# An attention stage in front of two feed-forward networks: four steps a pair, reciprocals through DRAM, weight preparation spread

## The reference

```python
def _attn_ref(q, k, v, M_prev, z_prev, beta):
    scores = scale * np.matmul(q, k.transpose(0, 1, 3, 2))
    scores = np.where(causal, -1000000000.0, scores)
    a = np.exp(scores - scores.max(-1, keepdims=True))
    a /= a.sum(-1, keepdims=True) + 1e-09
    local = np.matmul(a, v)
    q_p = phi(q)                       # where(q > 0, q, exp(q) - 1) + 1
    mem_ret = np.einsum('bhsd,bhde->bhse', q_p, M_prev)
    mem_norm = np.einsum('bhsd,bhd->bhs', q_p, z_prev)[..., None] + 1e-06
    g = 1.0 / (1.0 + np.exp(-beta))[None, :, None, None]
    return g * (mem_ret / mem_norm) + (1 - g) * local

x = (silu(x @ w_gate) * (x @ w_val)) @ w_out
h = x @ w_in
x = np.where(h >= 1, h, np.where(h <= -1, 0.0, (h + 1) ** 2 / 4)) @ w_out2
```

## Time and profile before

| | us |
|---|---|
| median of three runs | 1084.59 (1083.61 to 1087.66) |
| the profiled execution | 1084.93 |
| its span | 1083.0 |
| TensorE busy, share of the span | 1011.7, 93% |
| DVE, ACT, POOL busy | 817.6, 572.6, 535.4 |

### The profile page before, as it was taken

One profiled execution on the slowest core, in us unless ns is written; L12 is line 12 of the kernel. 1 busy time (PEld: TensorE's weight loads), 2 busy tenths in 40 slices (PEclk: granted clock), 3 DMA queues, 4 the chain that ended last, 5 costly groups with the idle time before them and its releaser, 6 DMA issues.

```text
span 1083.0 us, 21225 instructions
## 1 busy us (share of the span) xinstructions
PE 1011.7 (93%) x6440; PEld 931.9 (86%) x6440; DVE 817.6 (75%) x1580; ACT 572.6 (53%) x1162; POOL 535.4 (49%) x455
## 2 busy tenths in 40 slices
PE   4698999899899989999899999999999999999998
PEld 2466666667899979999899999999999999999997
DVE  4567777787677867677766777888898879987876
ACT  3556666776644544454534445554464554654551
POOL 4645555565875843235622347655744325523321
PEclk9889999999999999999999999999999999999999
DMA  4212333312433322342223322232331432234211
GB/s 156 75 56 88 94 94 94 94 46 79 156 117 125 110 98 98 116 137 79 98 98 119 116 98 98 98 117 92 104 117 63 172 118 91 85 117 142 92 40 59
DMA packets 47662, 109.56 MB, mean 101 GB/s; under 512 B 11360, under 2 KB 21600, under 8 KB 47584
## 3 DMA queue, kind: packets, MB, share of 16 engines
q1 hardware_dynamic: 47584, 108.56, 29.9%
HBM read 93.86 MB, written 14.68 MB: 100 GB/s over the span
## 4 chain that ended last, share of the span: by engine, by line
PE 77%; DVE 7%; issue 6%; ACT 3%; POOL 3%; DMA 2%; SPq 1%; DVEq 1%; ACTq 0%; POOLq 0%
PE ps L1325 22%; PE ps L1327 21%; PE ps L1326 21%; PE ps L1301 4%; PE ps L1253 4%; PE ps L1272 4%; DVE xt_l L1049 1%; ACT rown L721 1%; DVE xy L1135 1%; DVE hid_r L1125 1%; DVE tmp L1119 1%; DMA zb<-z 1%; PE ps L1294 1%; ACT wu_h L771 1%; DMA wu_r<-w_up 1%
## 5 line engine op out<-in xcount | busy, mean ns | idle before, releaser
L634 POOL TENSOR_TENSOR wu_l<-wu_r,wu_h 128x768 fp32r<-128x768 f32 (+1 forms) x75 | 140.6, 1883 | 394.1 <-ACT wu_h L771 394.0
L1325 PE MATMUL ps<-xt_h,wu_h 128*128 128x384 f32 x840 | 282.7, 337 | 16.9 <-DVE xt_l L1049 10.2
L1327 PE MATMUL ps<-xt_h,wu_l 128*128 128x384 f32 x840 | 280.8, 334 | 0.0
L1326 PE MATMUL ps<-xt_l,wu_h 128*128 128x384 f32 x840 | 280.8, 334 | 0.0
L1325 PE MATMUL ps<-hid_h,wd_h 128*128 128x384 f32 x672 | 226.7, 337 | 7.5 <-DVE xy L1135 7.3
L1327 PE MATMUL ps<-hid_h,wd_l 128*128 128x384 f32 x672 | 225.3, 335 | 0.0
L1326 PE MATMUL ps<-hid_l,wd_h 128*128 128x384 f32 x672 | 225.2, 335 | 0.0
L1135 DVE TENSOR_TENSOR xy<-xy,ps 128x384 f32<-128x384 f32 x288 | 157.5, 548 | 57.0 <-PE ps L1327 56.0
L830 ACT ACTIVATE hid_h<-hid_r 128x768 fp32r<-128x768 f32 x84 | 70.9, 844 | 209.1 <-DVE hid_r L1109 153.8
L1325 PEld LDWEIGHTS ps<-xt_h,wu_h 128*128 128x128 f32 x840 | 157.6, 188 | 23.9 <-issue 23.3
L1326 PEld LDWEIGHTS ps<-xt_l,wu_h 128*128 128x128 f32 x840 | 157.7, 188 | 0.0
(11 more groups left out here) (75 smaller groups left out, 1401.3 us busy)
## 6 DMA issues: line engine op xcount, KB each, us to landing
wu_r<-w_up SPq DMA_DIRECT2D x60, 512.0 KB, 4.7
wd_r<-w_down SPq DMA_DIRECT2D x42, 512.0 KB, 3.5
wu_r<-kept SPq DMA_DIRECT2D x38, 512.0 KB, 5.5
kept<-wu_r SPq DMA_DIRECT2D x19, 512.0 KB, 4.5
qk<-qT SPq DMA_DIRECT2D x16, 288.0 KB, 2.8
qk<-kT SPq DMA_DIRECT2D x16, 288.0 KB, 3.1
qn<-q_rest SPq DMA_DIRECT2D x16, 256.0 KB, 2.9
vm<-v_rest SPq DMA_DIRECT2D x16, 256.0 KB, 3.2
```

The lines of the kernel that those rows point to most:

```text
L634: nc.gpsimd.tensor_tensor(wu_l[u % 3][:, a:b], wu_r[u % 3][:, a:b], wu_h[u % 2][:, a - 1:b - 1].bitcast(F32), ALU.subtract).then_inc(low_p ...
L1325: nc.tensor.matmul(dst, w_hi, v_hi, start=start, stop=False, skip_group_check=onto)
L1326: nc.tensor.matmul(dst, w_hi, v_lo, start=False, stop=False, skip_group_check=onto)
L1327: return nc.tensor.matmul(dst, w_lo, v_hi, start=False, stop=stop, skip_group_check=onto)
```

## The change

- Tiles 1 to 4 come in the order 4, 3, 2, 1, four steps a pair. The first 64 queries of both heads are one tile of 128 rows: a block diagonal matrix of the queries, prepared ahead, gives their scores in one matmul over 128 rows (scores_f), with its own mask, maximum and exp, in the step of tile 1. The distances are now MEMS 1, TURN 3, VALUES 5, EVAC 6; ROWN, NEGS and PTS fall from 5 to 4.
- The reciprocals of a whole pair are one operation of nine columns (sums_inverse). SP writes them to the DRAM tensor rsums, turned (write_r), waits until they are there, and issues four reads that broadcast them over 64 partitions each (read_r). DVE multiplies from there in two pieces a pair. POOL's copies, TensorE's transposes and ACT's copies of reciprocals are gone.
- Three loads a pair in place of eight: qk_in (Q, K and the block diagonal), nat_in (q by rows, z beside it), vm_in (M_prev and V). qk_in of pair 0 is the first of all.
- No loop: all steps are written out, and no register is counted.
- wu_r2, wu_l2 and wu_h1 have a place of their own. The loads of weight steps 0 to 2 are issued at the start; their sums, high and low parts and the X parts stand at single steps of the attention (SUMS_AT and the tables beside it).
- The copies of groups to pt: one of nine is on DVE, before three of nine.

```diff
-    ROWN, NEGS, PTS = 5, 5, 5
+    EXP, MEMS, TURN, VALUES, EVAC = 1, 1, 3, 5, 6
+    ROWN, NEGS, PTS = 4, 4, 4
+    SUMS_AT, LOW_AT, HIGH_AT = (34, 38, 45), (42, 47), (38, 43)
+    KEEP = 11
+    X_SUMS_AT = (46, 48, 50, 52)
+    X_HIGH_AT = (48, 50, 52, 54, 56, 58, 60)
...
+            def write_r(p):
+                sp.wait_ge(rdend, p + 1)
+                sp.dma_start(rsums[p].rearrange("b p -> p b"), rden[:, p % 2], allow_slow_non_contiguous=True).then_inc(r_out, 16)
+
+            def read_r(p):
+                sp.wait_ge(r_out, 16 * (p + 1))
+                at_least(sp, x_done, 2 * (p - 1))
+                for h in range(2):
+                    half = slice(D * h, D * h + D)
+                    first = rsums[p, 0:1, half].broadcast_to([D, D])
+                    sp.dma_start(rbc[half, p % 2, 0:D], first).then_inc(r_in[p % 2], 16)
+                    rest = rsums[p, 1:].rearrange("(o i h) n -> o i h n", o=1, h=2)[:, :, h]
+                    sp.dma_start(rbc[half, p % 2, D:].rearrange("p (i n) -> p i n", n=P),
+                                 rest.broadcast_to([D, SLOTS, P])).then_inc(r_in[p % 2], 16)
...
+            for p in range(1, NPAIR):
+                if p + 1 < NPAIR:
+                    load_qk(p + 1)
+                    load_nat(p + 1)
+                write_r(p - 1)
+                if p > 1:
+                    load_v(p)
+                read_r(p - 1)
+                if p == KEEP:
+                    keep_sums(1)
...
+            def sums_inverse(p):
+                at_least(dve, expd, 2 * SLOTS * (p + 1))
+                at_least(dve, expdf, p + 1)
+                nc.vector.tensor_scalar(den[:, p % 2], rsum[:, p % 2], 1e-9, None, ALU.add).then_inc(dend, 1)
+                at_least(dve, dend, p + 1)
+                at_least(dve, r_out, 16 * (p - 1))
+                nc.vector.reciprocal(rden[:, p % 2], den[:, p % 2]).then_inc(rdend, 1)
...
             def out_x(j):
+                p, i = tile_of(j)
+                if i not in (3, 1):
+                    return
+                at_least(dve, pv_done, j + 1)
+                at_least(dve, r_in[p % 2], 64 * (p // 2 + 1))
+                dst, o, r = x_part(p, 0 if i == 3 else 1)
                 nc.vector.tensor_tensor(dst, o, r, ALU.mult).then_inc(x_done, 1)
...
+            def scores_f(j):
+                p, i = tile_of(j)
+                if i > 1:
+                    return
+                s = p % 2
+                at_least(pe, maxed, 2 * j - 1)
+                nc.tensor.matmul(psf[:, SCORE_F:SCORE_F + D], qk[:, s, 2 * S:], qk[:, s, S:S + D],
+                                 start=True, stop=True).then_inc(scoredf, 1)
```

More of the change, by code:

```diff
@@ L1163, in _ @@
                     add_down(n)
-                if 2 not in pieces_of_pool(u):
+                if u > 0 and 2 not in pieces_of_pool(u):
                     up_low(u + 1, 2)
@@ new lines, in values @@
+            def values(j):
+                p, i = tile_of(j)
+                s = p % 2
+                bank, col = out_place(i)
+                if i == 4:
+                    at_least(pe, v_scaled, p + 1)
+                    at_least(pe, x_done, 2 * p - 1)
+                if i == 2:
+                    at_least(pe, x_done, 2 * p)
+                for g in range(len(GROUPS[i])):
+                    pe.wait_ge(*copied(j, g))
+                if i == 1:
+                    for h in range(2):
+                        nc.tensor.matmul(ps[D * h:D * h + D, bank, 0:D], vm[:, s, h, 0], pt[:, j % PTS, 0, D * h:D * h + D],
+                                         start=True, stop=True)
@@ L1303, in values @@
                 mm.then_inc(pv_done, 1)
-            def body(it, first=False, drain=False):
-                for j in range(STEP):
-                    def due(back):
-                        return not (first and j < back) and not (drain and j >= back)
-                    if not drain:
-                        scores(it, j)
-                    if due(TURN):
-                        turn(it, j - TURN, (0, 1))
-                    if due(VALUES):
-                        values(it, j - VALUES)
-                    if due(TURN):
-                        turn(it, j - TURN, (2,))
@@ L1318, in _ @@
-            body(0, first=True)
-            with pe.Fori(1, ITS) as it:
-                body(it)
-            body(ITS, drain=True)
+            for j in range(NSTEP + VALUES):
+                if j < NSTEP:
+                    scores(j)
+                    scores_f(j)
+                if TURN <= j < NSTEP + TURN:
+                    turn(j - TURN, (0, 1))
+                if VALUES <= j:
+                    values(j - VALUES)
+                if TURN <= j < NSTEP + TURN:
+                    turn(j - TURN, (2,))
```

833 lines of the change are left out of this document (358 added, 475 removed).

## The result

The changed kernel takes **1164.01 us** (median of four runs, 1163.19 to 1167.55); the kernel before, run beside it, 1086.12 (1083.61 to 1090.15). The ratio is 1.072, with a 95% interval of 1.0677 to 1.0762: slower by 7.2%, where 1038.6 us and a gain were forecast. The second rival of the prediction came true, at a higher price than it had named.

What follows compares the result with a forecast made beforehand. TensorE was taken as nearly the bound of attention pairs (12.57 of 13.75 us busy). Attention 42.9 us shorter and 3.4 at the seam: 1084.9 - 42.9 - 3.4 = 1038.6 us; own range 1030 to 1046, 8 in 10: 1027 to 1064.

Steps and rivals of the forecast that it cites:

- Rival 2: Reciprocals' write: partial DRAM writes over 70 ns each make it slower than before; 1130 us at 110 ns; chance 0.07.
- the price of the write: Reciprocals' write to DRAM, 72 packets an engine: 3.3 us from below, 6.2 us at 49 ns a packet.
- L + 2.7 us: Least time of a pair: reciprocal to reads landed (L, middle 9.3 us) plus DVE's work behind it; 12.0 us.
- SP stands ready at the write: SP's queue at the reciprocals' write: loads ahead of it wait only for scores of the step before.
- weight pieces: Weight sums, copies and differences of steps 0 and 1, moved onto attention steps 34 to 50: 1.5 us cost.
- second maximum starts: Start of the kernel: the second tile's maximum begins at 15.4 us, not 18.70, 3.3 us earlier.
- from there to the last scores: Attention, second maximum to last scores: 15.5 pairs, 186.0 us, plus 1.5 for weight work.
- drain: Last five attention steps, from the last scores to the first feed-forward matmul: 10.5 us, 9.9 before.
- The seam: Passage from attention to feed-forward: 3.4 us of 4.8 us idle taken back, as three weight steps are already loaded and summed.
- The last pair: End of attention: its reciprocals and multiplies end some 2 us into feed-forward, covered by 3.2 us of products.
- wrong on L: Sign in the attention pairs: DVE idle ahead of its output multiply, reads as releaser, more than 1 us a pair.
- The sign of being right: Sign in the attention part: no TensorE idling over 2 us between 20 and 200 us, and a full clock there.

Runs made afterwards that it cites:

- opening DVE's circle alone: Output multiply one step later (EVAC 7 in place of 6), otherwise the changed kernel: 1137.42 us.
- the kernel without the way through DRAM: Changed kernel with no write or reads of reciprocals; DVE multiplies by a constant 1, so output is not divided by the sums: 1042.86 us.
- the fastest kernel (the natural q first): Changed kernel with reciprocals turned on TensorE, EVAC 7, transpose and copy later in their step, natural q loaded ahead of Q and K: 1040.96 us.
- the kernel with EVAC 7 and the transpose on TensorE: Changed kernel with reciprocals turned on TensorE, written as 9 rows of 512 bytes, and the output multiply one step later: 1048.35 us.

## Why the prediction was wrong

**The step that failed is the price of the write.** The prediction put a 4-byte packet at 9 to 49 ns, from a line through the earlier trace rows, and took 49 as the far end because those packets are 200 times as large. Measured, the write takes 10.4 us, and (10.4 - 2.7) / 72 = 107 ns, with the prediction's own 2.7 us for a small transfer and 72 packets an engine. The line itself was good: into SBUF, or 64 bytes apart, the write takes 2.4 to 4.0 us, which is 2.7 plus 0 to 18 ns a packet. What it could not hold was a cost of addresses, because its packets are runs of 909 and 3,642 bytes on average, and none of its rows has small writes side by side. A packet's size was the wrong axis: "200 times as large" sounded like a generous bound and bounded nothing. The text had "partial writes could cost more than any row shows", and then gave that 0.07.

**The formula held.** L + 2.7 us: L was 118.10 - 101.77 = 16.3 us, and from the reads' landing to the next reciprocal it took 2.4, together 18.7. Rival 2 put L at 15.2 for 110 ns a packet. The missing 1.1 us are SP's issue of the reads: 2.9 us from the first to the last (112.37 to 115.25) where 1.6 was taken from the 0.62 of the earlier trace rows; two of the four took over 1 us. Why is not shown.

**A circle was missed.** SP's queue was read as a list of what stands ahead of the write, and "SP stands ready at the write" was right. What stands behind the reads, the next pair's loads, was not followed to ACT and TensorE. This is why opening DVE's circle alone gives back only 27 us. That the mean period is 19.8 and not 18.7 us has mostly another reason: the two longest, 27.2 and 21.6 us, lie in the second half, where the weight pieces stand, and the other thirteen have a mean of 19.1.

**The rest of the sum**, by the kernel without the way through DRAM:

| term | forecast, us | without the way | changed kernel |
|---|---|---|---|
| second maximum starts | 15.4 | 15.22 | 14.78 |
| from there to the last scores | 187.5 | 189.9 | |
| drain | 10.5 | 10.4 | |
| first feed-forward matmul | 213.4 | 215.5 | 326.5 |
| span behind it | 823.3 | 825.1 | 836.3 |

The start and the drain were right. The pair was forecast at 11.9 without the circle and is 11.92. The weight pieces cost more: 15.5 pairs at 11.92 would be 184.8, so 5.1 us go to them and to the first pairs, not 1.5. The seam gave 1.6 us (826.7 to 825.1), not 3.4. Together these misses are 3.9 us, and the time without the way was 1042.86 against 1038.6, inside the forecast's own range.

**A wait behind the weight pieces** was overlooked too. The prediction priced the pieces by the room on POOL and DVE. In the fastest kernel (the natural q first) one period is 19.1 us where its neighbours are 12.2 and 13.3. SP's queue and DVE's timeline in it:

```profile
148.09 0.60 SPq L438 DMA_DIRECT2D kept<-wu_r  x1
...
151.93 0.69 DVE L929 TENSOR_TENSOR wu_l<-wu_r,wu_h 128x512 fp32r<-128x512 f32 x1 [6.87 <-issue]
```

DVE's low part of weight step 1 waits in the code until the step's sums are stored. SP issues that store only behind the reads of a pair, and it lands 3.8 us later; DVE idles 6.87 us, and TensorE 6.16 behind it. In the changed kernel the same wait is 11.30 us of DVE, within the longest period of 27.2 us. No run moved this store, so what it costs in all is not measured.

**The last pair.** The prediction had step 0's first three products cover it, and 1 to 3 us if that cover is gone. With a write of 10.15 us it cost 9.62 of idling, and TensorE came back at the lower of its two clocks, 1.2 GHz (granted 0.50 from 339.5 to 345.0 us, then 1.00), so that the part behind the seam is 836.3 - 825.1 = 11.2 us longer.

**Signs.** The prediction's "wrong on L" (DVE idle ahead of its multiply, with the reads as releaser) was met: 5.6 us a pair on average, in twelve pairs. The sign of being right, no idling of TensorE over 2 us and a full clock between 20 and 200 us, failed for the same reason.

## What to carry to other kernels

Where a transfer's form is in no row of the profile, its bound has to come from the property that is new in it (here: neighbouring 4-byte writes to DRAM), not from the nearest number. Turn on TensorE what has to be turned, and write whole rows: one transpose and one small copy a pair took 116 us off the changed kernel (1164.0 to 1048.3). And before a wait goes into an in-order queue, follow both what stands ahead of it and what stands behind it, up to the engine that comes round to the same wait again: each such circle is a lower bound of the period, and there may be two.

## What the runs showed that I had not expected

- 1,152 writes of 4 bytes to DRAM take from 3.1 to 43.7 us by their addresses; 4 bytes apart with rows 8,192 bytes apart is three to four times as slow as with rows 512 apart (32.4 to 43.7 against 9.8 to 11.5).
- A load issued behind such a write on the same queue lands behind it, not beside it: 384 KB in 14.4 us in place of 5.4, 4.9 us after the write was over (132.7 against 127.9); 320 KB of V in 11.8. Moving loads "into the shadow" of the write cost 149 us (1313.36 against 1164.01).
- In seven of the sixteen pairs of the changed kernel, SP took 1.0 to 1.6 us to issue one of the reads (as 1.22 at 112.86), and 0.6 or less for most others. In the kernel with EVAC 7 and the transpose on TensorE the median is 0.6 too, and the longest 1.31. What makes an issue slow is open.
